# Causal scores of a retention layer on the four quarters of the array, by half chunks

## Chip, cores and metric

One core of a Trainium2 chip runs the whole program. The metric is the device time of one execution in microseconds (us), the median of several executions.

## What is computed

Retention over q, k, v of shape (4, 8, 576, 64), in float32, followed by two dense layers over the 2304 tokens. Only the first part is touched:

```python
scores = scale * np.matmul(q, k.transpose(0, 1, 3, 2))
gamma = 1.0 - 2.0 ** (-5.0 - np.arange(H, dtype=np.float32))
rel = pos[:, None] - pos[None, :]
Dmat = np.where(rel >= 0, gamma[:, None, None] ** rel[None, :, :], 0.0)
ret = scores * Dmat[None, :, :, :]
return np.matmul(ret, v).astype(np.float32)
```

The first layer is h = x @ w_in (512 to 2048), a quadratic gate, g @ w_out (2048 to 512); the second is (x @ w_a) * (x @ w_b) (512 to 1536), then @ w_out.

## The kernel before

**Units.** Retention runs over 16 units (UNITS), each one batch and one pair of heads. A unit's 576 positions are four full chunks of 128 (FULL) and a tail of 64 (TAIL). Inside a chunk the scores are computed and weighted by a mask; what lies before the chunk comes in through a state of 64 x 64 per head, carried from chunk to chunk. The two heads of a pair lie on partitions 0 to 63 and 64 to 127.

**TensorE per unit n, in this order.** `scores(n)` (line 415): group 1 (the tail and chunks 3 and 2, into `score_b`), then group 0 (chunks 1 and 0, into `score_a`). For each chunk and head it is one matmul with 64 rows of contraction, the 128 keys of the chunk stationary and its 128 queries moving; the tail has 64 and 64. Both tensors have one PSUM bank for each head. The output has the keys on its partitions and the queries along the bank. `key_values(n)` (line 428): eight matmuls of 128 rows, 64 stationary and 64 moving columns, into `kv_b`. Then, for the unit before, `inner(n - 1)` (line 445, masked scores times v, 128 rows, 64 stationary columns) and `across(n - 1)` (line 459, state times decayed queries, 64 rows and 64 stationary columns), both into `ret_b`. Behind unit 15's scores and key-values and unit 14's inner and across comes `hidden(0, 0)` (lines 477 to 479), the first matmuls of the dense layer; it waits for unit 15's masked scores, since it writes the banks of `score_a`. Unit 15's inner and across follow it.

**The other engines per unit.** VectorE (DVE): `decay_mask(n)` multiplies the scores by the mask (lines 607, 609) into `probs`, `state_steps(n)` forms the states (621, 624). In units 8 to 11 it then takes a split of x (633), in units 13, 14 and 15 one of `w1` blocks 0, 1 and 2 (638), each behind a rounding by ScalarE (ACT, 830 and 834). ACT copies `ret_b` to `x_all` (818), and the rounding of `w1` block n - 13 stands ahead of the copy for unit n - 1. GpSimd (POOL): line 389 multiplies the keys by their decay, which `key_values(n)` waits for; lines 396 and 400 decay the queries, behind across of unit n - 2.

**Loads.** All on SyncE's queue: for each unit `kq` (keys and queries, features on partitions, 576 KB), `kvt` (keys and values, tokens on partitions, 512 KB), `vtail` (32 KB), into four slots (SLOTS). `kq` of unit n waits for the scores of unit n - 4, `kvt` for its inner. Behind units 0, 1 and 2 stands the table `decays` of the next pair, that of pair 0 is on ACT's queue. The table has for each pair of heads CONST = 2*128 + 128 + 2 + 1 = 387 floats per partition: mask, decay of the queries, decay of the keys, decay of a chunk. The sixteen blocks of `w1` (512 KB each) follow: block 0 behind unit 12, 1 to 9 behind unit 15, 10 to 15 when retention is done.

Of the kernel before, what the change touches and what calls it, by code (L numbers as in the profile page):

```python
# [24 lines left out]
ALU = mybir.AluOpType  # L25
# [4 lines left out]
P = 128  # L30
# [4 lines left out]
PAIRS = HEADS // 2  # L35
UNITS = BATCH * PAIRS
FULL = SEQ // P
TAIL = SEQ - FULL * P
# [22 lines left out]
SLOTS = 4  # L61
EARLY = 3
W1A = 10
MASKS = 2 * P
CONST = MASKS + P + 2 + 1

# [4 lines left out]
def build(nc, k_q, kv_tok, v_tail, w1, w2_ab, w2_out, decays_c, out):  # L73
    ctx = ExitStack()
    with ctx:
        def sem(name):
            return ctx.enter_context(nc.semaphore(name))

        def sb(name, shape, dt=F32, where=ctx):
            return where.enter_context(nc.sbuf_tensor(name, shape, dt))  # L80

        half = sb("half", [P, 2])
# [11 lines left out]
        with ExitStack() as first:  # L94
# [11 lines left out]
            with ExitStack() as s:  # L106
                kq = sb("kq", [P, SLOTS, 2, SEQ], F32, s)
# [3 lines left out]
                probs = sb("probs", [P, 2, 2, SEQ], F32, s)  # L111
                state = sb("state", [P, 2, FULL, HD], F32, s)
                decays = sb("decays", [P, PAIRS, CONST], F32, s)
            with ExitStack() as s:
# [33 lines left out]
        def ps(name, shape):  # L148
            return ctx.enter_context(nc.psum_tensor(name, shape, F32))

        score_a, score_b = ps("score_a", [P, 2, 512]), ps("score_b", [P, 2, 512])
# [20 lines left out]
        wo_loaded = [sem(f"wo_loaded{i}") for i in range(2)]  # L172
        halves_set = sem("halves_set")
        tails_zeroed = sem("tails_zeroed")
        keys_decayed = sem("keys_decayed")
        q_ready = sem("q_ready")
        scores_ready = sem("scores_ready")
        kv_ready = sem("kv_ready")
        probs_ready = sem("probs_ready")
# [53 lines left out]
        def groups(g):  # L233

            if g == 0:
                return [(0, P, 0), (1, P, P)]
            return [(2, P, 0), (3, P, P), (4, TAIL, 2 * P)]

        def width(g):
            return 2 * P if g == 0 else 2 * P + TAIL  # L240
# [14 lines left out]
        def o_rows(n):  # L255

            q, a = n // ROWS, n % ROWS
            at = (q // (NF2 // GROUP)) * SUPER + a * P
            return x_all[:, :, at:at + P]
# [26 lines left out]
        def scores_of(g):  # L286
            return score_a if g == 0 else score_b
# [90 lines left out]
        @block.gpsimd  # L378
        def _(pool):
            nc.gpsimd.memset(half[:, 0:1], 0.5).then_inc(halves_set, 1)  # L380
            nc.gpsimd.memset(half[:, 1:2], -0.5).then_inc(halves_set, 1)
            for n in range(UNITS):
                s, p, r = n % SLOTS, n % PAIRS, n // SLOTS + 1
                if n < PAIRS:
                    pool.wait_ge(decays_loaded[p], 16)
                pool.wait_ge(kvt_loaded[s], 16 * r)
                keys = kvt[:, s, 0, :, :].rearrange("p c (h d) -> p c h d", h=2)
                kdec = decays[:, p:p + 1, MASKS + P:MASKS + P + 2]
                nc.gpsimd.tensor_tensor(keys, keys, kdec.unsqueeze(3).to_broadcast([P, FULL, 2, HD]),
                                        ALU.mult).then_inc(keys_decayed, 1)  # L390
                pool.wait_ge(kq_loaded[s], 16 * r)
                if n >= 2:
                    pool.wait_ge(ret_ready, 2 * (n - 1))

                qdec = decays[:, p, MASKS:MASKS + P]
                nc.gpsimd.tensor_tensor(
                    qd[:, n % 2, P:FULL * P].rearrange("p (c i) -> p c i", c=FULL - 1),
                    kq[:, s, 1, P:FULL * P].rearrange("p (c i) -> p c i", c=FULL - 1),
                    qdec.unsqueeze(1).to_broadcast([P, FULL - 1, P]), ALU.mult)
                nc.gpsimd.tensor_tensor(qd[:, n % 2, FULL * P:], kq[:, s, 1, FULL * P:],  # L400
                                        qdec[:, 0:TAIL], ALU.mult).then_inc(q_ready, 1)

        @block.tensor
        def _(pe):
            def scores(n):
                s = n % SLOTS
                pe.wait_ge(kq_loaded[s], 16 * (n // SLOTS + 1))
                for g in (1, 0):
                    if n:
                        pe.wait_ge(probs_ready, 3 * (n - 1) + (3 if g == 0 else 2))  # L410

                    for c, ln, at in reversed(groups(g)):
                        for head in range(2):
                            dims = slice(head * HD, (head + 1) * HD)
                            mm = pe.matmul(scores_of(g)[0:ln, head, at:at + ln],
                                           kq[dims, s, 0, c * P:c * P + ln],
                                           kq[dims, s, 1, c * P:c * P + ln], start=True, stop=True)
                    mm.then_inc(scores_ready, 1)

            def key_values(n):  # L420
# [11 lines left out]
            def inner(n):  # L432
                s = n % SLOTS
                pe.wait_ge(vtail_loaded[s], 16 * (n // SLOTS + 1))
                if n == 0:
                    pe.wait_ge(tails_zeroed, 2)
                pe.wait_ge(probs_ready, 3 * n + 3)
                for g in range(2):
                    if n:
                        pe.wait_ge(ret_copied, 2 * (n - 1) + g + 1)  # L440
                    for c, ln, at in groups(g):
                        for head in range(2):
                            dims = slice(head * HD, (head + 1) * HD)
                            v = kvt[:, s, 1, c, dims] if c < FULL else vtail[:, s, dims]
                            mm = pe.matmul(ret_b[g][dims, at:at + ln], v,
                                           probs[:, n % 2, head, c * P:c * P + ln],
                                           start=(at == 0), stop=(c == 0), skip_group_check=True)
                mm.then_inc(inner_done, 1)
# [51 lines left out]
            for n in range(UNITS):  # L500
                scores(n)
                key_values(n)
                if n:
                    inner(n - 1)
                    across(n - 1)
# [88 lines left out]
        def _(dve):  # L594
            def decay_mask(n):
                p = n % PAIRS
                if n < PAIRS:
                    dve.wait_ge(decays_loaded[p], 16)
                mask = decays[:, p, 0:MASKS].rearrange("p (h i) -> p h i", h=2)
                for g in (1, 0):  # L600
                    dve.wait_ge(scores_ready, 2 * n + 2 - g)
                    if n >= 2:
                        dve.wait_ge(inner_done, n - 1)
                    o = probs[:, n % 2, :, 2 * g * P:2 * (g + 1) * P].rearrange("p h (c i) -> p h c i", c=2)
                    i = scores_of(g)[:, :, 0:2 * P].rearrange("p h (c i) -> p h c i", c=2)
                    m = mask.unsqueeze(2).to_broadcast([P, 2, 2, P])
                    nc.vector.tensor_tensor(o, i, m, ALU.mult).then_inc(probs_ready, 1)
                    if g:
                        nc.vector.tensor_tensor(probs[0:TAIL, n % 2, :, FULL * P:],
                                                score_b[0:TAIL, :, 2 * P:2 * P + TAIL],  # L610
                                                mask[0:TAIL, :, 0:TAIL], ALU.mult).then_inc(probs_ready, 1)

            def state_steps(n):
# [4 lines left out]
                for c in range(FULL):  # L618
# [3 lines left out]
                    else:  # L622
                        dve.wait_ge(state_ready, FULL * n + c)
                        nc.vector.scalar_tensor_tensor(
                            out=state[:, n % 2, c, :], in0=state[:, n % 2, c - 1, :],
                            scalar=decays[:, p, CONST - 1:CONST], in1=kv, op0=ALU.mult,
                            op1=ALU.add).then_inc(state_ready, 1)
# [61 lines left out]
            def add_rows(step, place):  # L689
                for n in shares_ended(step, place):  # L690
                    if not first_share(n):
                        dve.wait_ge(rows_done, n + 1)
                        nc.vector.tensor_tensor(o_rows(n), y_b[n % 4].rearrange("p (k i) -> p k i", k=KT),
                                                o_rows(n), ALU.add).then_inc(rows_out[n % 4], 1)


            nc.vector.memset(vtail[TAIL:, :, :], 0.0).then_inc(tails_zeroed, 1)
            nc.vector.memset(probs[TAIL:, :, :, FULL * P:], 0.0).then_inc(tails_zeroed, 1)
# [277 lines left out]
def constants():  # L976
    heads = np.arange(HEADS, dtype=np.float32)
    gamma = (1.0 - 2.0 ** (-5.0 - heads)).astype(np.float64)
    pos = np.arange(P, dtype=np.float64)

    rel = pos.reshape(1, 1, 1, P) - pos.reshape(P, 1, 1, 1)
    mask = np.where(rel >= 0, gamma.reshape(1, PAIRS, 2, 1) ** np.maximum(rel, 0), 0.0) / np.sqrt(HD)
    rows = np.repeat(gamma.reshape(PAIRS, 2), HD, axis=1).T
    qdec = rows[:, :, None] ** pos[None, None, :] / np.sqrt(HD)
    kdec = gamma.reshape(1, PAIRS, 2) ** (P - pos)[:, None, None]
    gchunk = rows[:, :, None] ** P
    return np.concatenate([mask.reshape(P, PAIRS, MASKS), qdec, kdec, gchunk], axis=2).astype(np.float32)


# [42 lines left out]
```

## Time and profile before

| | us |
|---|---|
| median of 3 executions | 881.88 (881.67 to 882.44) |
| the profiled execution | 882.61 |
| its span, first to last instruction | 880.1 |
| PE busy | 870.2 (99%) |
| DVE busy | 479.8 (55%) |
| ACT busy | 334.6 (38%) |
| POOL busy | 37.0 (4%) |

PE stands for TensorE's matmuls, PEld for its weight loads, which run beside them. A profile page begins with the busy time of each engine and then cuts the span into 40 slices of 22 us, one digit each, the busy share in tenths. In a timeline, a row is a run of like instructions: start, time from the first one's start to the last one's end, engine, line, operation, output and input, rows*columns of the stationary operand for PE, shapes, count, and in brackets how long the engine had been idle and what ended that. A matmul's own duration contains its way through the array; several lie over each other, so their pace is read from the spacing of the starts: (length of the row - duration of one) / steps. Retention lies in the first 70 us or so.

### The profile page before, as it was taken

How to read it: one execution, taken by the hardware profiler on the slowest of the kernel's cores; microseconds unless marked ns; L12 is line 12 of the kernel's file. 1: busy time of each engine (PE TensorE's matmuls, PEld its weight loads, DVE VectorE, ACT ScalarE, POOL GpSimd, SP SyncE). 2: the span in 40 equal slices, each digit the busy share in tenths (PEclk: the TensorE clock that was granted, in tenths of full speed). 3: DMA queues.
4: the chain of work that ended last, by engine and by line, in shares of the span. 5: the costliest groups of instructions: out<-in, count | busy, mean ns of one | idle time of the engine just before them, and what ended most of it. 6: DMA issues, size and time to landing. Idle time of an engine off the chain costs nothing.

```text
span 880.1 us, 13001 instructions
## 1 busy us (share of the span) xinstructions
PE 870.2 (99%) x5232; PEld 777.0 (88%) x5232; DVE 479.8 (55%) x829; ACT 334.6 (38%) x598; POOL 37.0 (4%) x54
## 2 busy tenths in 40 slices
PE   7999999999999999999999999999999999999998
PEld 6998888888899888888889999999999999999996
DVE  4686665555656755665653533574433574534443
ACT  1235554444445544444443333342233242223220
POOL 4660000000000000000000000000000000000000
PEclk9999999999999999999999999999999999999999
DMA  9996000223232123222335644545454845454622
GB/s 344 329 348 264 1 0 1 79 111 116 111 123 108 54 107 119 111 112 105 118 149 189 243 168 184 198 157 200 150 198 157 284 159 215 168 216 168 227 60 72
DMA packets 33451, 136.89 MB, mean 156 GB/s; under 512 B 2672, under 2 KB 13424, under 8 KB 28784
## 3 DMA queue, kind: packets, MB, share of 16 engines
q1 hardware_dynamic: 33248, 135.87, 42.0%
q8 instruction: 41, 0.67, 0.3%
q10 hardware_dynamic: 144, 0.20, 0.1%
q14 instruction: 18, 0.15, 0.0%
HBM read 109.32 MB, written 26.74 MB: 155 GB/s over the span
## 4 chain that ended last, share of the span: by engine, by line
PE 97%; DMA 1%; SPq 1%; DVE 0%; ACT 0%; issue 0%; POOL 0%; POOLq 0%; DVEq 0%; ACTq 0%
PE score_b L523 6%; PE score_b L527 6%; PE score_b L525 6%; PE score_a L527 4%; PE score_a L523 4%; PE score_a L525 4%; PE score_a L477 4%; PE kv_b L494 4%; PE kv_b L496 4%; PE score_a L479 4%; PE ret_b L496 4%; PE score_b L479 4%; PE score_a L478 4%; PE kv_b L495 4%; PE score_b L477 4%; PE ret_b L495 4%
## 5 line engine op out<-in xcount | busy, mean ns | idle before, releaser
L717 DVE TENSOR_TENSOR gate_w<-relu_s,relu_r 128x512 f32<-128x512 f32 (+1 forms) x80 | 51.0, 638 | 97.2 <-ACT relu_r L895 97.1
L523 PE MATMUL score_b<-xop_hi,wop 128*128 128x384 f32 x288 | 96.8, 336 | 0.1
L527 PE MATMUL score_b<-xop_hi,wop 128*128 128x384 f32 x288 | 96.7, 336 | 0.0
L525 PE MATMUL score_b<-xop_lo,wop 128*128 128x384 f32 x288 | 96.5, 335 | 0.0
L904 ACT ACTIVATE gh<-gated 128x512 fp32r<-128x512 f32 (+1 forms) x80 | 47.2, 590 | 105.9 <-DVE gated L720 105.9
L726 DVE TENSOR_TENSOR gl<-gated,gh 128x512 fp32r<-128x512 f32 (+1 forms) x80 | 51.1, 639 | 50.8 <-ACT gh L904 50.6
L523 PE MATMUL score_a<-xop_hi,wop 128*128 128x384 f32 x216 | 72.2, 334 | 0.0
L527 PE MATMUL score_a<-xop_hi,wop 128*128 128x384 f32 x216 | 72.2, 334 | 0.0
L525 PE MATMUL score_a<-xop_lo,wop 128*128 128x384 f32 x216 | 72.2, 334 | 0.0
L954 ACT ACTIVATE p<-score_b 128x384 f32<-128x384 f32 x36 | 17.7, 490 | 105.3 <-PE score_b L527 105.3
L523 PEld LDWEIGHTS score_b<-xop_hi,wop 128*128 128x128 f32 x288 | 54.1, 188 | 2.0 <-ACT p L954 0.4
L946 ACT ACTIVATE ph<-prod 128x384 fp32r<-128x384 f32 x36 | 18.9, 526 | 96.4 <-DVE prod L763 96.4
L525 PEld LDWEIGHTS score_b<-xop_lo,wop 128*128 128x128 f32 x288 | 54.1, 188 | 1.3
L527 PEld LDWEIGHTS score_b<-xop_hi,wop 128*128 128x128 f32 x288 | 54.0, 188 | 0.0
L720 DVE SCALAR_TENSOR_TENSOR gated<-relu_s,gate_w 128x512 f32<-128x512 f32 (+1 forms) x80 | 51.1, 638 | 2.7
L781 DVE TENSOR_TENSOR prod<-score_a,a 128x384 f32<-128x384 f32 x18 | 10.0, 557 | 72.6 <-PE score_a L527 72.6
L893 ACT ACTIVATE relu_s<-score_a,half 128x512 f32<-128x512 f32 (+1 forms) x40 | 25.8, 646 | 55.4 <-PE score_a L479 55.4
L781 DVE TENSOR_TENSOR prod<-score_b,a 128x384 f32<-128x384 f32 x18 | 10.0, 557 | 64.5 <-PE score_b L527 64.5
L477 PE MATMUL score_a<-xh,w1a 128*128 128x512 f32 (+1 forms) x120 | 44.4, 370 | 0.0
L478 PE MATMUL score_a<-xl,w1a 128*128 128x512 f32 (+1 forms) x120 | 44.2, 368 | 0.0
L479 PE MATMUL score_a<-xh,w1a 128*128 128x512 f32 (+1 forms) x120 | 44.1, 368 | 0.0
L548 PE MATMUL kv_b<-wo_hi,pl 128*128 128x512 f32 x112 | 43.9, 392 | 0.0
(129 smaller groups left out, 2144.1 us busy)
## 6 DMA issues: line engine op xcount, KB each, us to landing
wop<-w_ops SPq DMA_DIRECT2D x36, 1792.0 KB, 7.2
w_ops<-op_hi SPq DMA_DIRECT2D x12, 896.0 KB, 4.7
w_ops<-op_lo SPq DMA_DIRECT2D x12, 896.0 KB, 6.5
kq<-k_q SPq DMA_DIRECT2D x16, 576.0 KB, 6.2
wo_raw<-w_out SPq DMA_DIRECT2D x9, 1024.0 KB, 9.6
kvt<-kv_tok SPq DMA_DIRECT2D x16, 512.0 KB, 5.7
ab_raw<-w_ab SPq DMA_DIRECT2D x12, 512.0 KB, 3.7
w1a_raw<-w SPq DMA_DIRECT2D x10, 512.0 KB, 10.1
```

The costliest lines, as they stand in the source:

```text
L477: pe.matmul(o, w1_slab(f, 0)[:, at], xh[:, k, 0:WIDTHS[t]], start=(k == 0), stop=False)
L478: pe.matmul(o, w1_slab(f, 0)[:, at], xl[:, k, 0:WIDTHS[t]], start=False, stop=False)
L479: mm = pe.matmul(o, w1_slab(f, 1)[:, at], xh[:, k, 0:WIDTHS[t]], start=False, stop=(k == KT - 1))
L495: pe.matmul(o, w1_slab(f, 0)[:, at], gl[:, f % RING, 0:WIDTHS[t]], start=False, stop=False)
L496: mm = pe.matmul(o, w1_slab(f, 1)[:, at], gh[:, f % RING, 0:WIDTHS[t]], start=False, stop=(f == NF1 - 1))
L523: pe.matmul(o, w[:, 0, at], xop_hi[b][:, k, :], start=(start and k == 0), stop=False, skip_group_check=True)
L525: pe.matmul(o, w[:, 0, at], xop_lo[b][:, k, :], start=False, stop=False, skip_group_check=True)
L527: mm = pe.matmul(o, w[:, 1, at], xop_hi[b][:, k, :], start=False, stop=(k == 1), skip_group_check=True)
L717: nc.vector.tensor_tensor(gate_w[:, 0:WIDTHS[t]], relu_s[:, 0:WIDTHS[t]], relu_r[:, 0:WIDTHS[t]], ALU.add).then_inc(gatew_ready, 1)
L720: nc.vector.scalar_tensor_tensor(out=gated[:, 0:WIDTHS[t]], in0=relu_s[:, 0:WIDTHS[t]], scalar=1.0, in1=gate_w[:, 0:WIDTHS[t]], op0=ALU.mi ...
L726: nc.vector.tensor_tensor(gl[:, f % RING, 0:WIDTHS[t]], gated[:, 0:WIDTHS[t]], raw(gh[:, f % RING, 0:WIDTHS[t]]), ALU.subtract).then_inc(g ...
L904: nc.scalar.activation(gh[:, f % RING, 0:WIDTHS[t]], gated[:, 0:WIDTHS[t]], ACT.Copy).then_inc(gh_ready, 1)
```

## The change

The scores of a chunk are computed by halves of 64 keys. The first half meets all 128 queries of the chunk, the second half only the last 64, for the quarter of the square that is left has all its keys behind its queries and is masked out. So each chunk and head has a matmul of 64 stationary and 128 moving columns and one of 64 and 64. A half goes to output partitions 0 to 63 or 64 to 127; in odd chunks the two halves change places (`half_at`), so that the four matmuls of two neighbouring chunks and two heads lie on four different quarters of the array: row half by head, column half by chunk. The order in a group is: the tail (group 1), then the first halves of both chunks, then the second halves of both.

Since the keys of odd chunks now lie swapped on the partitions of the scores, the host swaps the halves of odd chunks in `kvt` (keys and values), and the table holds the mask a second time with its halves swapped and a key decay for each chunk: 4*128 + 128 + 8 + 1 = 649 floats per partition and pair. VectorE's mask product takes the doubled mask as it lies, without a broadcast over chunks. The part of `score_a` and `score_b` that no matmul writes any more is zeroed once at the start by two memsets on VectorE, for which the first scores and the first mask product wait.

```diff
-MASKS = 2 * P
-CONST = MASKS + P + 2 + 1
+HP = P // 2
+MASKS = 4 * P
+KDEC = MASKS + P
+CONST = KDEC + 2 * FULL + 1
@@
+        def half_at(c, half):
+            return HP * (half ^ (c % 2))
@@ (GpSimd)
-                kdec = decays[:, p:p + 1, MASKS + P:MASKS + P + 2]
+                kdec = decays[:, p, KDEC:KDEC + 2 * FULL].rearrange("p (c h) -> p c h", c=FULL)
@@ (TensorE)
+                if n == 0:
+                    pe.wait_ge(scores_zeroed, 2)
                 for g in (1, 0):
                     if n:
                         pe.wait_ge(probs_ready, 3 * (n - 1) + (3 if g == 0 else 2))
-                    for c, ln, at in reversed(groups(g)):
+                    def part(c, half, at, ln):
+                        rows, first = slice(half_at(c, half), half_at(c, half) + HP), c * P + half * HP
                         for head in range(2):
                             dims = slice(head * HD, (head + 1) * HD)
-                            mm = pe.matmul(scores_of(g)[0:ln, head, at:at + ln],
-                                           kq[dims, s, 0, c * P:c * P + ln],
-                                           kq[dims, s, 1, c * P:c * P + ln], start=True, stop=True)
+                            mm = pe.matmul(scores_of(g)[rows, head, at + half * HP:at + half * HP + ln],
+                                           kq[dims, s, 0, first:first + HP], kq[dims, s, 1, first:first + ln],
+                                           start=True, stop=True)
+                        return mm
+                    if g:
+                        part(FULL, 0, 2 * P, TAIL)
+                    for half in range(2):
+                        for c, ln, at in groups(g)[:2]:
+                            mm = part(c, half, at, P - half * HP)
                     mm.then_inc(scores_ready, 1)
@@ (VectorE)
+                if n == 0:
+                    dve.wait_ge(scores_zeroed, 2)
-                    o = probs[:, n % 2, :, 2 * g * P:2 * (g + 1) * P].rearrange("p h (c i) -> p h c i", c=2)
-                    i = scores_of(g)[:, :, 0:2 * P].rearrange("p h (c i) -> p h c i", c=2)
-                    m = mask.unsqueeze(2).to_broadcast([P, 2, 2, P])
-                    nc.vector.tensor_tensor(o, i, m, ALU.mult).then_inc(probs_ready, 1)
+                    nc.vector.tensor_tensor(probs[:, n % 2, :, 2 * g * P:2 * (g + 1) * P],
+                                            scores_of(g)[:, :, 0:2 * P], mask,
+                                            ALU.mult).then_inc(probs_ready, 1)
@@
+            nc.vector.memset(score_b[:, :, 0:2 * P], 0.0).then_inc(scores_zeroed, 1)
+            nc.vector.memset(score_a[:, :, 0:2 * P], 0.0).then_inc(scores_zeroed, 1)
@@ (host)
+    mask = np.stack([mask, halves_swapped(mask, 0)], axis=3)
+    kdec = np.stack([halves_swapped(kdec, 0) if c % 2 else kdec for c in range(FULL)], axis=2)
@@
-        return token_major(a)[:, :FULL * P].reshape(UNITS, FULL, P, P).transpose(0, 2, 1, 3)
+        chunks = token_major(a)[:, :FULL * P].reshape(UNITS, FULL, P, P)
+        chunks = [halves_swapped(chunks[:, c], 1) if c % 2 else chunks[:, c] for c in range(FULL)]
+        return np.stack(chunks, axis=2)
```

## Rows read from the trace of the kernel before

**Rows 1.** The page: busy time of the engines, and the chain's shares.

```profile
PE 870.2 (99%) x5232; PEld 777.0 (88%) x5232; DVE 479.8 (55%) x829; ACT 334.6 (38%) x598; POOL 37.0 (4%) x54
...
PE 97%; DMA 1%; SPq 1%; DVE 0%; ACT 0%; issue 0%; POOL 0%; POOLq 0%; DVEq 0%; ACTq 0%
```

**Rows 2.** Waits, 0 to 92 us: us in total, times, longest us.

```profile
PE score_b L415 <- DMA kq<-k_q: 5.6, 1, 5.6
...
POOL kvt L389 <- DMA kvt<-kv_tok: 13.2, 7, 6.3
...
PEld kv_b L428 <- POOL kvt L389: 1.2, 3, 0.5
```

**Rows 3.** DMA, 0 to 80 us in 40 slices of 2 us; the table's queue.

```profile
DMA  1899999999999997899899899999998999953999
GB/s 25 261 409 400 381 399 364 405 362 378 398 374 362 387 308 249 293 364 312 312 336 320 294 340 333 380 385 363 312 282 310 420 404 420 416 207 55 367 416 416
...
q10 hardware_dynamic: 144, 0.20, 0.8%
```

**Rows 4.** Timeline, 30 to 42 us: one steady unit, PE and PEld.

```profile
33.40 0.92 PE L415 MATMUL score_b<-kq 64*64 64x64 f32 x11
...
34.16 0.61 PE L415 MATMUL score_a<-kq 64*128 64x128 f32 x8
...
34.70 0.55 PEld L428 LDWEIGHTS kv_b<-kvt 128*64 128x64 f32 x16
...
35.21 1.05 PE L445 MATMUL ret_b<-probs,kvt 128*64 128x128 f32 x16
...
37.02 0.27 PE L415 MATMUL score_b<-kq 64*64 64x64 f32 x1
37.02 0.27 PE L459 MATMUL ret_b<-qd,state 64*64 64x64 f32 x3
...
37.12 0.92 PE L415 MATMUL score_b<-kq 64*64 64x64 f32 x11
```

**Rows 5.** Timelines from 0 and (Pool's) from 18 us: key products, one key-value run.

```profile
7.12 1.04 POOL L389 TENSOR_TENSOR kvt<-kvt,decays 128x512 f32<-128x512 f32 x1 [6.26 <-DMA kvt<-kv_tok]
...
14.22 1.04 POOL L389 TENSOR_TENSOR kvt<-kvt,decays 128x512 f32<-128x512 f32 x1 [1.22 <-DMA kvt<-kv_tok]
...
18.71 1.04 POOL L389 TENSOR_TENSOR kvt<-kvt,decays 128x512 f32<-128x512 f32 x1 [2.38 <-DMA kvt<-kv_tok]
...
19.81 0.69 PE L428 MATMUL kv_b<-kvt 128*64 128x64 f32 x16 [0.27 <-POOL kvt L389]
...
21.67 1.04 POOL L389 TENSOR_TENSOR kvt<-kvt,decays 128x512 f32<-128x512 f32 x1 [0.84 <-DMA kvt<-kv_tok]
...
24.68 1.06 POOL L389 TENSOR_TENSOR kvt<-kvt,decays 128x512 f32<-128x512 f32 x1 [0.73 <-DMA kvt<-kv_tok]
...
28.03 1.04 POOL L389 TENSOR_TENSOR kvt<-kvt,decays 128x512 f32<-128x512 f32 x1 [0.47 <-DMA kvt<-kv_tok]
```

**Rows 6.** Single lines' instructions, 33 to 37 us: duration ns min/median/max.

```profile
L415 PE MATMUL score_a<-kq x8: 272/272/272, 34.2 to 34.5; 64*128 64x128 f32 x8
...
L428 PEld LDWEIGHTS kv_b<-kvt x16: 132/138/138, 34.7 to 35.1; 128*64 128x64 f32 x16
```

**Rows 7.** Timeline, 44 to 82 us: where retention ends.

```profile
45.54 0.69 DVE L607 TENSOR_TENSOR probs<-score_b,decays 128x512 f32<-128x512 f32 x1 [0.57 <-PE score_b L415]
...
62.17 1.06 ACT L834 ACTIVATE w1a<-w1a_raw 128x1024 fp32r<-128x1024 f32 x1 [2.06 <-DMA w1a_raw<-w]
...
63.13 0.70 ACT L818 ACTIVATE x_all<-ret_b 128x256 f32<-128x256 f32 x2
...
65.00 1.22 PE L445 MATMUL ret_b<-probs,kvt 128*64 128x128 f32 x15
...
65.20 0.67 DVE L607 TENSOR_TENSOR probs<-score_a,decays 128x512 f32<-128x512 f32 x1
...
67.30 0.50 PE L477 MATMUL score_a<-xh,w1a 128*128 128x512 f32 x1
```

More of the change, by code:

```diff
@@ L174, in build @@
         tails_zeroed = sem("tails_zeroed")
+        scores_zeroed = sem("scores_zeroed")
         keys_decayed = sem("keys_decayed")
@@ L985, in constants, with halves_swapped @@
     kdec = gamma.reshape(1, PAIRS, 2) ** (P - pos)[:, None, None]
+    kdec = np.stack([halves_swapped(kdec, 0) if c % 2 else kdec for c in range(FULL)], axis=2)
     gchunk = rows[:, :, None] ** P
-    return np.concatenate([mask.reshape(P, PAIRS, MASKS), qdec, kdec, gchunk], axis=2).astype(np.float32)
+    parts = [mask.reshape(P, PAIRS, MASKS), qdec, kdec.reshape(P, PAIRS, 2 * FULL), gchunk]
+    return np.concatenate(parts, axis=2).astype(np.float32)
+def halves_swapped(a, axis):
+    return np.roll(a, HP, axis=axis)
 def kernel(q, k, v, moe_w_in, moe_w_out, moe2_w_a, moe2_w_b, moe2_w_out):
```

## The prediction

> **What bounds the kernel now.** I read the page first: TensorE (PE) is busy 870.2 of 880.1 us and carries 97% of the chain [rows 1]. So time is won only where PE's own work shrinks, and only if nothing else then holds PE. The list of waits of the first 92 us, in which all of retention lies, says how far away the others are: PE waits 5.6 us for the first `kq`, and PE's weight loads wait only 1.2 us for Pool's decayed keys. Pool itself waits 13.2 us for `kvt` transfers [rows 2]. The two-microsecond slices show why: the DMA moves 360 to 400 GB/s from the fourth microsecond on and its share stands at nine tenths nearly throughout retention [rows 3]. So two resources lie close together: PE needs 3.72 us per unit (the tail's scores start at 33.40 and at 37.12) [rows 4], and the DMA brought the `kvt` of units 4 and 5 3.01 us apart [rows 5].
>
> **Part 1, scores on four quarters.** A float32 matmul leaves two records (`score_a` in one unit: 4 matmuls, x8) [rows 6]. The eight `score_a` records, 0.27 each, start over 0.61 - 0.27 = 0.34 us, three steps of 0.113: two records (two heads) per step, for 128 moving columns. The key-value records, 64 moving columns, take (0.55 - 0.14) / 7 = 0.059 per pair of weight loads; 128 columns behind 64 stationary ones (inner) take (1.05 - 0.27) / 7 = 0.111 per pair [rows 4, 6].
> Before, from the tail's start at 33.40 to `score_a` at 34.16 is 0.76: tail 2 x 0.059 = 0.12, chunks 4 x 0.113 = 0.45, and 0.19 left over. From 34.16 to the inner matmuls at 35.21 is 1.05: 4 x 0.113 + 8 x 0.059 = 0.92, leaving 0.13. From 35.21 to 37.12 is 1.91: inner 8 x 0.111 + 2 x 0.059, across 6 x 0.111 + 2 x 0.059 = 1.79, leaving 0.12. These three remainders stand exactly where the shape on the array changes (64x64 to 64x128, 64x128 to 128x64, 128x64 to 64x64); between across and the tail's scores, both 64x64, there is none, and one tail record even starts together with the last across records, at 37.02 [rows 4]. I price a change of shape at 0.19 for the one that goes.
> The Trainium skill (TensorEngine Tiling (Array Packing), Key Properties) says that changing the tiling mode, unlike changing the tile, drains the engine. The remainders agree.
> After, all scores are 64x64, so the change between the tail and the chunks goes: -0.19. Per group a chunk is one half of 128 columns and one of 64, and two chunks x two heads fill four quarters. If four records go side by side at the pace at which two do, a group takes 2 x 0.111 + 2 x 0.059 = 0.34 instead of 0.45: -0.11, twice per unit. Sum 0.19 + 0.22 = 0.41 per unit; I take 0.40.
> What speaks for four at once: at 37.02 a record of `score_b` (row half 64, column half 0) starts beside across records on the two diagonal quarters, so three quarters run together (the quarters of the across heads are taken, the record can only be the tail's other head), and a later instruction overtakes earlier ones of an occupied quarter [rows 4]. Each head writes its own bank, as before.
> From the other side: instructions. The scores go from 10 matmuls (20 records) to 18 (36). The closest spacing held over a stretch is the key-value one, 0.029 per record; at that pace 36 records take 1.06 against 0.79 by columns, and the saving shrinks to 0.12 + 0.90 + 0.19 - 1.06 = 0.15 per unit. The bounds of part 1 by these rows are 0.15 and 0.42, and a loss only by the mechanism under rivals.
>
> **Part 2, the table of decays grows** from 387 to 649 floats per partition: a head pair's transfer from 198 to 332 KB. Pair 0's goes on ACT's queue, 1 to 3 stand on SP's queue, each ahead of its unit's `kq` and `kvt`. All four lie before unit 3's keys. The landings show the price: Pool starts on units 0 and 2 at 7.12 and 14.22, 3.55 per unit (with a table of 198 KB), on 4 and 5 at 21.67 and 24.68, 3.01 apart (without) [rows 5]. So 198 KB cost 0.54, and 134 KB more 0.36; by the bytes of table queue 10 (0.20 MB in 0.8% of 80 us) [rows 3] it is 0.43, at the 380 GB/s of the slices 0.35. Four times: +1.4 us (1.2 to 1.7) on the landing of unit 3's keys, 18.71 -> 20.1; Pool's product takes 1.04, so its key-value matmuls start at 21.2 instead of 19.81 [rows 5]. PE comes earlier than that (unit 2's keys land at about 15.2, kv at 16.3, plus 3.3), so the saving of the first units is lost in this wait and +1.4 stands. Bounds: 1.0 (if the table rows move better in longer pieces) and 1.8.
> Does it go on? Unit 4's keys land at 21.67 + 1.4 = 23.1, ready at 24.2, while PE wants them at 21.2 + 3.32 = 24.5; unit 5's ready at 27.2, wanted at 27.8. From there PE leads again, each key transfer is sent when the unit four before it is through (SP), and at 3.32 us per unit the DMA must move 576 + 512 + 32 KB (1.147 MB), 345 GB/s, below the 380 of the slices. Cover is thin, not gone.
>
> **Part 3, small things.** Two memsets of PSUM on DVE ahead of the others stand where nothing else is queued but the two memsets of before; even at 1 us each (a 128x512 product with a PSUM operand takes 0.69 [rows 7]) they end before the first `kq` lands at 5.6 [rows 2], for which PE and, behind it, DVE wait anyway: 0. DVE's mask product loses its broadcast, same 512 elements per partition, 0.69: 0 +- 0.05, and even in a unit with a split DVE sits idle 0.57 us ahead of it [rows 7]. Pool's key product reads its factor from other addresses: 0. The swapped halves are made on the host: 0.
>
> **Part 4, what meets the earlier PE at the end.** Nothing ahead of unit 15 waits on `w1`, but on ACT the rounding of `w1` block 1 stands before the copy that frees `ret_b` for inner of unit 14, and on DVE its split stands before unit 15's mask, on which the first hidden matmul waits. The transfer landed at 62.17; ACT's copy began at 63.13, was through at about 63.5 (half of the row's 0.70) for inner at 65.00, the mask ended at 65.20 + 0.67 = 65.87 for hidden at 67.30: 1.4 us of slack [rows 7]. PE will be there 12 x 0.40 - 1.4 = 3.4 us earlier; the transfer is sent behind unit 15's keys, which wait for inner of unit 11, some 9 x 0.40 - 1.4 = 2.2 earlier. Slack left 0.2, and the DMA is asked for more per us in units 12 to 15 (one `w1` block beside them). I take +0.4 (0 to 1.5). Later nothing: hidden needs a new block only every 24 matmuls, and they arrive in a row.
>
> **Sum.** 12 steps from unit 3 to unit 15 x -0.40 = -4.8; +1.4; +0.4: **-3.0 us**. The profiled run was 882.61 (span 880.1), it would become 879.6; the median of the runs 881.88 becomes **878.9**.
>
> **Rivals.**
> B, instruction pace. Quarters overlap, but records come no faster than 0.029 each: 0.15 per unit, 12 x 0.15 = 1.8, less 1.4, and no squeeze at the end: 881.5. For it: nothing in retention is issued faster over a stretch. Against: PE's queue has slow stretches (across, inner) in which to get ahead, and starts a few ns apart occur.
> The Trainium skill (TensorE: Matmul & The Clock Gate, "Wait - 56ns, not 53.3ns?") gives some 62 ns of sequencer work per matmul where it is not decoded in hardware. Eighteen matmuls would be 1.12 us, a saving of 0.09 per unit and no gain in total; the rows' eight key-value matmuls in 0.47 us, 59 ns each, don't exclude it.
> C, the DMA becomes the bound: the keys land every 3.5 us instead of 3.3, as between units 2 and 6 (14.22 to 28.03, 3.45 each) [rows 5]. Then 12 x 0.22 - 1.4 = 1.2: 880.7.
> D, slower: not more than two score records run at a time (two streams for the same rows, or weight loads of the second column half waiting). A group is then 4 x 0.111 + 4 x 0.059 = 0.68 instead of 0.45, 0.46 more per unit, less 0.19: 12 x 0.27 + 1.4 = +4.6: 886.5. With -0.19 for the change of shape, the kernel gets slower once a group takes over 0.49 us, by 0.2% at 0.56. Against it: the three at 37.02.
> E, the table costs more than its bytes (a 2.5 us hole before unit 3) with part 1 as forecast: 4.8 - 2.5 - 0.4 = 1.9: 880.0.
>
> **Chances.** Forecast (878 to 880) 0.5, B 0.17, C 0.13, E 0.08, D 0.12. A change under 0.2% (1.8 us) can't be told from none: faster (below 880.1) is the forecast and most of E, some of C: 0.6; same 0.28 (B, most of C); slower 0.12 (D). Range 877.3 (part 1 at its full 0.42 and the lower bounds of the delays: -5.0 + 1.0 = -4.0, and a little) to 882.3 (B with the upper bound of the table); D is left out.
>
> **What would show it.** `score_a` and `score_b` as 64x64 records, four within about 0.03 us, `score_b` to `score_a` near 0.46 and a unit at 3.32 us in the thirties; Pool's product of unit 3 starting near 20.1; PE waiting for it about 1.5 us; the first hidden matmul near 64.3. Wrong if units stay above 3.5 us with PE busy (B, D), if Pool waits for `kvt` beyond unit 6 with PE behind it (C), or if unit 3's keys land as early as before.

## The result and the profile after

| | before | after |
|---|---|---|
| median, us | 881.88 | 886.08 |
| range of the runs (5 each) | 881.52 to 882.73 | 885.97 to 887.3 |
| ratio, 95% interval | | 1.0048 (1.0036 to 1.0059) |
| span of the profiled execution | 880.1 | 884.1 |
| PE busy | 870.2 | 866.7 |

The change makes the kernel 4.2 us slower, while PE is busy 3.5 us less. The page's line of the instruction queue has two fetches more than before (41 there):

```profile
PE 866.7 (98%) x5488; PEld 774.3 (88%) x5488; DVE 481.0 (54%) x831; ACT 334.8 (38%) x598; POOL 36.7 (4%) x54
...
q8 instruction: 43, 0.70, 0.3%
```

The timeline from 30 to 42 us, the stretch of [rows 4], PE alone. Columns as there: start, length, engine, line, operation; in brackets the idle time and what ended it.

```profile
34.47 0.27 PE L426 MATMUL score_b<-kq 64*64 64x64 f32 x1
34.47 0.27 PE L477 MATMUL ret_b<-qd,state 64*64 64x64 f32 x3
...
34.58 0.56 PE L426 MATMUL score_b<-kq 64*64 64x64 f32 x18
...
34.98 0.55 PE L426 MATMUL score_a<-kq 64*64 64x128 f32 x15
...
35.46 0.69 PE L446 MATMUL kv_b<-kvt 128*64 128x64 f32 x16
...
35.97 1.05 PE L463 MATMUL ret_b<-probs,kvt 128*64 128x128 f32 x16
...
37.88 0.56 PE L426 MATMUL score_b<-kq 64*64 64x64 f32 x18
...
38.76 0.69 PE L446 MATMUL kv_b<-kvt 128*64 128x64 f32 x16
...
40.97 1.09 PE L463 MATMUL ret_b<-probs,kvt 128*64 128x128 f32 x16 [1.52 <-issue]
```

The first unit is what part 1 forecast: 34.58 to 37.88 is 3.30 us instead of 3.72. The scores take 0.40 from `score_b` to `score_a` and 0.48 from there to the key-value matmuls, which with 0.13 for the change of shape in it is 0.35 for a group. Fifteen `score_a` records start within 0.55 - 0.22 = 0.33 us, 0.024 apart. So four quarters do work at once. The next unit has a hole: the key-value matmuls start at 38.76, the inner ones not 0.51 later but at 40.97, and what ended the wait is "issue", no engine and no data.

The list of waits, 0 to 92 us, has these lines (before, PE's only wait for issue was 0.5 us on weight loads):

```profile
POOL kvt L396 <- DMA kvt<-kv_tok: 12.5, 7, 6.3
...
PE ret_b L463 <- issue: 3.6, 3, 1.6
...
PE kv_b L446 <- POOL kvt L396: 1.5, 2, 0.8
PE kv_b L446 <- issue: 1.5, 1, 1.5
...
PE score_a L426 <- issue: 1.0, 2, 0.7
```

The start and the end of retention, to be read beside [rows 5] and [rows 7], from the timelines from 0, from 48 and from 60 us:

```profile
11.99 1.12 PE L446 MATMUL kv_b<-kvt 128*64 128x64 f32 x16 [0.79 <-POOL kvt L396]
...
12.90 1.92 PE L463 MATMUL ret_b<-probs,kvt 128*64 128x128 f32 x16
...
14.61 1.04 POOL L396 TENSOR_TENSOR kvt<-kvt,decays 128x512 f32<-128x512 f32 x1 [1.59 <-DMA kvt<-kv_tok]
...
17.43 0.69 PE L446 MATMUL kv_b<-kvt 128*64 128x64 f32 x16
...
19.37 1.05 POOL L396 TENSOR_TENSOR kvt<-kvt,decays 128x512 f32<-128x512 f32 x1 [1.38 <-DMA kvt<-kv_tok]
...
20.73 0.69 PE L446 MATMUL kv_b<-kvt 128*64 128x64 f32 x16
...
24.32 0.34 PE L426 MATMUL score_a<-kq 64*64 64x64 f32 x7 [0.32 <-issue]
...
52.23 0.62 PE L446 MATMUL kv_b<-kvt 128*64 128x64 f32 x14 [1.49 <-issue]
...
62.98 0.55 PE L426 MATMUL score_a<-kq 64*64 64x128 f32 x11 [0.71 <-issue]
...
66.76 0.69 PE L446 MATMUL kv_b<-kvt 128*64 128x64 f32 x16
...
69.67 0.54 PE L463 MATMUL ret_b<-probs,kvt 128*64 128x128 f32 x5 [1.58 <-issue]
...
71.28 0.50 PE L495 MATMUL score_a<-xh,w1a 128*128 128x512 f32 x1
```

**Where the 4.0 us of the span come from.** Unit 3's key-value matmuls start at 20.73 instead of 19.81: +0.9. Twelve units of 3.30 instead of 3.72: -5.0. But from 20.73 to unit 15's at 66.76 it is 46.0 and not 39.6: +6.4. From there to the first hidden matmul it is 4.52 instead of 2.81: +1.7. Sum +4.0, and hidden starts at 71.28 instead of 67.30. After that the two kernels run alike.

**What the +0.9 consists of.** Unit 3's keys land 0.66 us later and are ready at 19.37 + 1.05 = 20.42. Its key-value matmuls start at 20.73 without a wait: 3.30 us behind unit 2's at 17.43. So here PE came last, by 0.3 us, and not the keys. PE was late because it ran slowly until 16.6 us: unit 0's inner matmuls (12.90) take 1.92 us, in the kernel before 1.04 (at 12.54). The trace's first record of a full granted clock stands at 16.60, before at 12.31. The same rows with the same lengths (1.12 and 1.92) come back once in the run phase below, from 70.55 on, where the profile gives a granted clock of 0.50. Ahead of 16.60 PE had waited 0.75 and 0.79 us for keys. Other runs have this first record between 9.17 and 15.57, and why it comes late in one and early in another is open.

**What the holes have in common.** I counted PE's records (weight loads, matmuls, waits) in the order of their starts, and took the packets of queue 8 from the trace, each 16,384 bytes, 256 instructions of 64 bytes. Every hole of the changed kernel from unit 4 on lies right behind record 705, 961, 1473, 1985, 2497 or 2753, all 193 plus a multiple of 256:

```
records   start of   packet that brings   from the start of
before    the next   the next block       the record before
          one, us    (start to end)       to this start, us
 705      24.32      21.78 to 22.81       0.54
 961      29.98      27.39 to 28.46       0.81
1217      34.86      31.57 to 33.15       0.00
1473      40.97      38.68 to 39.65       1.74
1729      46.17      43.06 to 44.07       0.00
1985      52.23      49.97 to 50.93       1.72
2241      57.53      55.19 to 56.30       0.29
2497      62.98      60.40 to 61.42       0.98
2753      69.67      67.16 to 68.10       1.85
```

Where there is a hole, PE goes on 1.2 to 1.6 us after the packet's end. This holds for all eleven traces of this case, the runs below included: between 12 and 75 us no block starts sooner than 1.23 us after the end of its packet, and the 25 gaps of over 0.2 us at block starts all end 1.23 to 1.58 us after it.

Two things differ from the kernel before. Its blocks last 6.5 us (33.30 to 39.71 to 46.22) and none runs dry; a unit has 36 matmuls of four records and some waits before, 44 after, in less time, so a block lasts some 4.7 us. And the packets wait longer now. From the moment a block is entered to the start of the packet for the next one it was 2.6, 1.9, 1.6, 0.8, 0.5 and 4.3 us before (blocks entered from 27.04 to 59.13), and 3.1, 1.6, 3.8, 2.1, 3.8, 3.0 and 2.9 after (24.32 to 57.53). The 4.3 shows how near the kernel before already was to a hole: the packet for the block that starts at 65.74 ran from 63.41 to 64.40, 1.34 before it.

### The profile page after: what moved, and what is told of

It is laid out like the page before. It is cut to its first block, busy times and chain, and to the rows that moved or that the text cites. A ratio compares the mean times of both kernels' runs of the same rounds, so it can differ in the third digit from the quotient of the medians.

```text
span 884.1 us, 13516 instructions
## 1 busy us (share of the span) xinstructions
PE 866.7 (98%) x5488; PEld 774.3 (88%) x5488; DVE 481.0 (54%) x831; ACT 334.8 (38%) x598; POOL 36.7 (4%) x54
## 4 chain that ended last, share of the span: by engine, by line
PE 97%; DMA 1%; issue 1%; SPq 0%; DVE 0%; ACT 0%; POOL 0%; DVEq 0%; ACTq 0%; POOLq 0%
PE score_b L541 6%; PE score_b L545 6%; PE score_b L543 6%; PE score_a L545 4%; PE score_a L543 4%; PE score_a L541 4%; PE score_a L495 4%; PE kv_b L512 4%; PE score_b L495 4%; PE ret_b L512 4%; PE score_a L497 4%; PE score_a L496 4%; PE kv_b L513 4%; PE kv_b L514 4%; PE score_b L496 4%; PE ret_b L513 4%
```

## The experiments

**Theory F**: PE runs out of instructions. A block of 256 is asked for when the one before it is entered; the packet waits beside the transfers of `kq` and `kvt`, which keep the DMA nine tenths busy, and a block now lasts less long than that takes. **Rival G**: instructions come at a pace of their own, whatever the data do. **Rival H**: it has nothing to do with counts; the quarters or a semaphore hold PE.

### Less data, the same instructions: light_loads

```diff
+                w = SEQ if n < SLOTS else P
-                sp.dma_start(kq[:, s, :, :], k_q[n]).then_inc(kq_loaded[s], 16)
+                sp.dma_start(kq[:, s, :, 0:w], k_q[n][:, :, 0:w]).then_inc(kq_loaded[s], 16)
+                c = FULL if n < SLOTS else 1
-                sp.dma_start(kvt[:, s, :, :, :], kv_tok[n]).then_inc(kvt_loaded[s], 16)
+                sp.dma_start(kvt[:, s, :, 0:c, :], kv_tok[n][:, :, 0:c, :]).then_inc(kvt_loaded[s], 16)
```

> The changed kernel, with the transfers of kq and kvt for units 4 to 15 cut to 128 of 576 positions and to one chunk of four (the rest of a slot keeps an older unit's numbers, so those units are not computed rightly); all instructions of all engines stay. Theory F (PE runs out of instructions: their fetches, 256 instructions each, queue behind the data transfers of retention): the holes of 0.4 to 1.7 us in PE at every 256th instruction go between units 4 and 12, units take 3.30 us there, and only the two holes beside the w1 blocks (62.98 and 69.67) may stay; 8.1 us of holes become 0 to 2.6, so 886.1 becomes 878 to 881. Theory G (instructions come at a fixed pace, whatever the data traffic; 45 more of them per us is too many): the holes stay, 886. Theory H (the quarters themselves or a semaphore hold PE): the holes stay, 886.

Measured: 879.23, ratio to before 0.997 (0.9959 to 0.9981), 6.9 us below the changed kernel. Its DMA line from 24 to 56 us, and PE's key-value matmuls from its timeline of PE:

```profile
DMA  5420643051515224535042503406998416410575
...
24.02 0.69 PE L448 MATMUL kv_b<-kvt 128*64 128x64 f32 x16
27.32 0.69 PE L448 MATMUL kv_b<-kvt 128*64 128x64 f32 x16
30.62 0.69 PE L448 MATMUL kv_b<-kvt 128*64 128x64 f32 x16
33.92 0.69 PE L448 MATMUL kv_b<-kvt 128*64 128x64 f32 x16
...
57.04 0.69 PE L448 MATMUL kv_b<-kvt 128*64 128x64 f32 x16
60.34 0.69 PE L448 MATMUL kv_b<-kvt 128*64 128x64 f32 x16
62.55 0.54 PE L465 MATMUL ret_b<-probs,kvt 128*64 128x128 f32 x5 [0.88 <-issue]
```

Twelve units of 3.30 us in a row, with all instructions. The packets of the blocks entered at 28.49, 33.33, 37.69, 42.90 and 47.19 start 0.9, 0.1, 0.6, 0.4 and 1.5 us later; in the changed kernel, between 29.98 and 57.53, it was 1.6, 3.8, 2.1, 3.8, 3.0 and 2.9. The one hole left is at record 2753, beside the `w1` blocks (its packet started 3.7 us after the block was entered). G and H fall: the instructions, the quarters and the semaphores are the same here, and 3.30 us per unit is kept up. What it doesn't show alone is that the boundaries of blocks are the places; the next run does.

### The blocks shifted: phase

```diff
+            for i in range(128):
+                pe.wait_ge(scores_zeroed if i % 2 else halves_set, 1)
             for n in range(UNITS):
                 scores(n)
```

> The changed kernel with 128 waits that are long met ahead of PE's first scores, while PE waits for the first kq anyway. They become some 64 to 127 more instructions. Theory F and G: holes stand at every 256th instruction of PE, so in the program they come 64 to 127 instructions earlier, at other matmuls than before (so far unit 4's score_a, units 6, 9, 12 and 14, behind the 705th, 961st, 1473rd, 1985th, 2497th and 2753rd instruction); counted with the added ones they stand at the same numbers. The sum of the holes may change by some us either way. Theory H: the holes stay at the same matmuls. Time within 883 to 889 by all.

The 128 waits became 64 instructions (two conditions in each). Holes over 0.2 us stood behind records 449 (0.80), 705 (0.40), 961 (2.35), 1473 (0.27), 1729 (2.07), 2241 (1.74) and 2753 (2.93): at the same numbers, 64 instructions earlier in the program. The one at 961 was in inner of unit 4 in the changed kernel, and is now in the last records of the scores of a unit (timeline of PE, 26 to 31 us):

```profile
27.21 0.55 PE L426 MATMUL score_a<-kq 64*64 64x128 f32 x14
29.89 0.27 PE L426 MATMUL score_a<-kq 64*64 64x64 f32 x1 [2.13 <-issue]
30.09 0.69 PE L446 MATMUL kv_b<-kvt 128*64 128x64 f32 x16
```

The one run took 888.97, within the expectation of 883 to 889: another phase, other holes, in sum more. About 1 us of it is not the holes themselves: PE stood from 67.4 to 70.13, the granted clock fell from 1.0 to 0.5 (to 1.2 GHz) at 69.88 and rose again at 73.29, and from unit 15's key-value matmuls to hidden it took 3.80 us instead of 2.81. The waits also held PE's first scores until 8.47 instead of 5.78, and unit 3's key-value matmuls still started at 20.62. Here the clock was full from 11.85, PE came early and waited 0.71 us for unit 3's keys, so in this run their landing decided.

### The w1 blocks later: w1_late

```diff
-            for f in range(1, W1A):
-                load_w1(f)
+            load_w1(1)
+            load_w1(2)
+            sp.wait_ge(ret_ready, 2 * UNITS - 2)
+            for f in range(3, W1A):
+                load_w1(f)
```

> The changed kernel with w1 blocks 3 to 9 sent when unit 14 is through, instead of behind unit 15's keys; nothing computed changes. Theory F: the hole of 1.85 us at 69.67, whose fetch ran from 67.16 beside these transfers, shrinks to under 0.5; the one at 62.98 (0.98) may shrink. 886.1 becomes 883.5 to 884.7. Theories G and H: no change, 886.

Measured: 885.2 (882.45 to 887.34, 6 runs), 1.0031 (1.0015 to 1.0048). The hole at record 2753 is gone (its packet ran from 63.85 to 64.82, PE got there at 66.14) and with it most of the 1.7 us; the only wait for issue after unit 12 is this one, from its timeline of PE, 64 to 70 us:

```profile
65.66 1.13 PE L466 MATMUL ret_b<-probs,kvt 128*64 128x128 f32 x16
...
66.84 0.99 PE L480 MATMUL ret_b<-qd,state 64*64 64x128 f32 x16
68.18 0.47 PE L498 MATMUL score_a<-xh,w1a 128*128 128x512 f32 x1 [0.35 <-issue]
```

The holes at 961, 1473 and 1985 stayed, 1.63, 0.65 and 1.60 in the profiled run. The median lies a little above what was expected and the runs spread by 5 us; that the packets' waits differ from one execution to the next would explain it, but one execution alone was profiled. The medians (885.2 against 886.08) would not carry F.

The 0.35 us at 68.18 does not stand at a block's start. VectorE's mask product for unit 15 (`probs<-score_a`, 67.40, 0.67 us long) ends at 68.07 there, since the 2.05 us split of a `w1` block (64.63) stood ahead of it on VectorE. Hidden waits for this mask: it is the wait that part 4 of the prediction named, and it cost about 0.2 us (3.03 from unit 15's key-value matmuls instead of 2.81).

### The table alone: big_table

```diff
-CONST = MASKS + P + 2 + 1
+CONST = MASKS + P + 2 + 1 + 262
```

> The kernel before, with 262 unused floats added to each partition's table of a head pair, so that it is as long as in the changed kernel. The prediction's part 2 said +1.4 us (bounds 1.0 and 1.8): 883.3. The trace of the changed kernel shows its unit 3 keys landing 0.66 us later (19.37 instead of 18.71), which would make +0.6 to +0.7: 882.5. If the fetches of instructions are slowed by it too, holes appear in PE as well, and it is more.

Measured: 882.87, 1.0012 (1.0003 to 1.0022): +1.0 us. In its timeline unit 3's keys come at 19.61 and its key-value matmuls at 20.89, in the kernel before 18.71 and 19.81:

```profile
19.61 1.06 POOL L389 TENSOR_TENSOR kvt<-kvt,decays 128x512 f32<-128x512 f32 x1 [2.29 <-DMA kvt<-kv_tok]
20.89 0.69 PE L428 MATMUL kv_b<-kvt 128*64 128x64 f32 x16
```

So the landing moves 0.9, PE 1.1, and hidden 0.8 (68.09). PE was 0.2 us behind the keys here too (ready at 20.67; unit 2's key-value matmuls at 17.17 plus 3.72 is 20.89; full clock from 15.37). 134 KB more per unit cost 0.9 / 4 = 0.23 us of landing, less than in proportion to the 0.54 that the first 198 KB seemed to cost. No holes appeared; 3.72 us per unit throughout.

### More instructions in the old scores: more_instructions

```diff
+            def met_waits():
+                pe.wait_ge(tails_zeroed, 1)
+                pe.wait_ge(halves_set, 1)
@@ ahead of each matmul of retention
+                            met_waits()
```

> The kernel before, with its old scores, and ahead of each of a unit's 36 matmuls two waits that are long met: about 36 more instructions of PE per unit, 183 in place of 147, and the same work for the array. Theory F: 256 instructions now last 5.2 us instead of 6.5, less than the 6 to 7 us that a fetch takes from the moment its predecessor is entered; holes of 1 to 2 us appear at every 256th instruction, 4 to 9 us in sum, 886 to 891. Theory H (the holes belong to the quarters): no holes; the units stay at 3.72 us, or all get longer by the same amount if PE's sequencer can't keep up with the waits, at most 1.8 us each.

Inconclusive. The time was 902.62 (one run), a unit took 5.2 us, evenly: 576 met waits (36 in a unit) cost 1.5 us per unit, 0.04 each. So 256 instructions lasted 7 us and there was nothing to see at their boundaries; the largest gap there was 0.13 us. F's figure of 886 to 891 was wrong because I had taken the added instructions as free, and the result is what H allowed in its second branch. A kernel with the old scores and blocks of under 5 us was not measured.

### Fewer transfers under way: capped

As w1_late, and:

```diff
                 if n >= SLOTS:
+                    sp.wait_ge(kvt_loaded[(n - 1) % SLOTS], 16 * ((n - 1) // SLOTS + 1))
                     sp.wait_ge(scores_ready, 2 * (n - SLOTS) + 2)
```

> As w1_late, and kq of a unit from the fourth on is only sent when kvt of the unit before has landed, so that at most one unit's transfers stand ahead of a fetch of instructions. Theory F: fetches start within 2 us instead of 3 to 4 after they are due, the holes at 30, 40 and 52 us shrink below 0.5 each; if the DMA then has pauses, Pool waits for keys instead. 881 to 883, against 885 of w1_late. Theory G: the holes stay, 885.

Measured: 906.82, 1.0285 (1.027 to 1.0301), 25 us slower than before. No wait for issue stood in retention up to 80 us, but PE waited for keys:

```profile
DMA  0469775008999207899508499800999950539992
...
POOL kvt L400 <- DMA kvt<-kv_tok: 47.6, 15, 6.2
...
PE kv_b L450 <- POOL kvt L400: 16.3, 11, 2.6
```

The DMA (24 to 56 us) now has pauses, a unit takes 5 to 6 us. The expectation was off by twenty-odd us: with transfers that take 3.7 (`kq`) and 4.8 us (`kvt`) from issue to landing there, a stream of 3.3 us per unit needs more than one unit under way. The granted clock fell to 0.5 three times as well, for 3.4 us each (from 32.63, 63.35 and 80.42). About F this run says nothing: its blocks lasted 6.5 to 9.1 us between 23.66 and 78.01, as long as in the kernel before or longer.

### The quarters in every other unit, in the last eight, in the last four

every_other is w1_late with the following; even units have the matmuls of the kernel before, and its order of halves on the host:

```diff
                         for c, ln, at in groups(g)[:2]:
+                            if n % 2:
                                 mm = part(c, half, at, P - half * HP)
...
```

> As w1_late, with the quarters in odd units alone; even units have the old scores of 128 keys, and the old order of halves in kvt, mask and key decay. Theory F: a pair of units takes 3.30 + 3.72, and 256 instructions last 5.5 us, nearer to what a fetch takes: holes 0 to 3 us in sum instead of 5, the saving 6 x 0.42 = 2.5 instead of 5.0; 881 to 883. Theory H (the quarters as such): holes only in odd units, 883 to 885.

last_four and last_eight have `n >= Q0` in that place, with Q0 = 12 and 8, and load the table's added part later (at n == 3 in last_eight):

```diff
+                if n == 7:
+                    sp.dma_start(decays[:, :, LATE:], decays_c[:, :, LATE:]).then_inc(late_loaded, 16)
```

> The quarters in units 12 to 15 alone, with the order of halves in kvt, mask and key decay switched there too; the second half of the table (1056 bytes per partition and pair) is sent in one transfer behind unit 7, so the start has the old table of 198 KB; w1 blocks 3 to 9 wait until unit 14 is through, as in w1_late. Theory F: units 12 to 15 meet a DMA that is running empty, so 256 instructions may last less than 5 us there without a hole; 4 x 0.42 = 1.7 us saved, the start as in the kernel before: 880.2 (879.8 to 881). Theory G (a fixed pace of instructions): a hole of 1 to 2 us in units 12 to 15, 881.5 to 882.

> The same from unit 8 on, the second half of the table behind unit 3. Theory F: units 8 to 11 run beside the full DMA, where a fetch takes 6 to 7 us from the moment it is due; 8 x 0.42 = 3.4 us less, one or two holes of 1 to 1.7 us between 40 and 56 us: 879.5 to 881.5. Theory G: three or four holes, 882 to 884.

| | median, us | ratio to before | units after unit 3, us |
|---|---|---|---|
| every_other | 881.74 | 1.0 (0.9991 to 1.001) | 3.72 / 3.30 in turn, once 3.84, 4.14 and 4.49 |
| last_four | 881.6 | 0.9997 (0.9987 to 1.0006) | 3.72, then 3.30, 3.30, 3.30, 4.76 |
| last_eight | 882.74 | 1.0006 (0.9997 to 1.0015) | 3.72, then 3.30, 3.30, 3.69, 3.30, 4.68, 4.09, 3.62, 3.30; unit 4 4.36 |

(The last column is from the starts of the key-value matmuls.) None beats the kernel before by what can be told. The quarters save their 0.42 in each unit that has them, and block boundaries take it back. every_other came out as F expected. last_four (881.6) and last_eight (882.74) did not: both lie where their expectations put theory G, with the hole or holes that it named. It is light_loads that rules G out, not these two; what they show is that I had set the packets' waits too short.

In last_four, where the start has the old table and unit 3's matmuls start at 19.35, one hole remains (timeline of PE from 59 us):

```profile
60.65 0.98 PE L501 MATMUL ret_b<-qd,state 64*64 64x128 f32 x15
62.74 0.21 PE L501 MATMUL ret_b<-qd,state 64*64 64x64 f32 x1 [1.12 <-issue]
```

Its packet ran from 60.28 to 61.30 though its predecessor was entered at 56.14. The claim in its expectation that units 12 to 15 meet a DMA running empty was wrong: the keys of unit 15 and two `w1` blocks were still on their way. In every_other 256 instructions last some 5.5 us (two units have 328 in 3.72 + 3.30); one hole of 1.24 us was left, at record 1985, and one of 0.38 at 1473. In last_eight they are 0.33, 1.33 and 0.84, at 1473, 1729 and 1985.

## Why the prediction was wrong

Forecast 878.9, range 877.3 to 882.3, "faster" 0.6. Measured 886.08.

- **Part 1 (0.40 per unit)** was right, mechanism and size: 3.30 us where 3.32 was said, a group 0.35 where 0.34, the change of shape gone. Twelve units bring 5.0.
- **Part 2 (+1.4 at unit 3)** was mis-sized: the keys landed 0.66 us later in the changed kernel and 0.9 in big_table. The step "so 198 KB cost 0.54, and 134 KB more 0.36" took the cost as proportional to bytes; it measured 0.17 and 0.23. PE's key-value matmuls moved 0.9 and 1.1, since "PE comes earlier than that" failed in these two profiles: PE, at the lower clock until 16.60 and 15.37, came 0.3 and 0.2 us after the keys. In phase, w1_late and light_loads it came early and waited for them, as said. The clock was in no term.
- **Part 2, "Does it go on?"** asked only whether data come in time. They did (Pool waited as long for `kvt`, 12.5 instead of 13.2). It didn't ask what else uses the same DMA. Its 380 GB/s is the rate of the first 28 us; from 28 to 60 us [rows 3] has 249 to 385.
- **The step that failed** is the one that priced the added instructions, "From the other side: instructions". It asked how fast PE can issue them and bounded that by the key-value spacing. It never asked how they come to PE. 256 more matmul records and as many weight loads are two more packets in retention, and each packet has to arrive in 4.7 instead of 6.5 us, and the packets also started later than before. That is 6.4 + 1.7 = 8.1 us of holes (with small shifts in between; the seven gaps of the list alone are 7.9), which no term and no rival had. Why the packets started later, and why by so unequal times, is open. The page showed the queue (q8, 41 packets), and the number of records per packet could have been had from it, roughly: 10,464 matmuls and weight loads in 41 packets is 255, PE's own waits not counted.
- **Part 4 (+0.4)** was not put to the test in the changed kernel: PE came late, not early, to the end of retention. In w1_late its mechanism shows, with about 0.2 us.
- **Part 3** cost nothing, as said: two memsets of 0.48 us each, done at 1.94; the mask product 0.69 as before.
- **Rivals.** D had nearly the measured time (886.5) and is still wrong: its mechanism, that no more than two records run at a time, is refuted by the 3.30 us. B (pace of issue) stood closest in subject, but light_loads issues the same instructions at 3.30 us per unit, and the eighteen score matmuls take 0.88 us (34.58 to 35.46), under B's 1.06 and under the 1.12 named beside it. C, the DMA as the bound, was right that the full DMA is where the gain goes, and wrong about which transfers suffer.

The Trainium skill (Runtime: NRT & Kernel Launch, Instruction fetch mechanics) says that each engine's instructions are refilled in 16 KiB blocks of 256, the next while the current one runs, and that the cost of crossing a boundary is mostly hidden. The trace agrees on size and place. On the cost it agrees for the kernel before and for light_loads (with the one hole named), not for the changed kernel, where the boundaries cost 8.1 us; here the measurement decides.

## What to carry to other kernels

More and smaller instructions on PE have a price that no busy share shows: each 256 of them are a 16 KB transfer that shares the DMA with the data. Before splitting matmuls in a stretch where the DMA is nine tenths busy, divide 256 by the instructions per us of that stretch and compare with the time from entering a block to the end of the next one's packet, plus the 1.2 to 1.6 us that follow; here 6.5 us was just enough and 4.7 was not. The faster kernel's packets waited longer, so a figure from the kernel before is a lower bound. In a trace, waits for "issue" at distances of 256 or 512 records are this; one that stands elsewhere (w1_late at 68.18) is not.

## What the runs showed of the hardware that I had not expected

- Four 64x64 quarters of the array took float32 matmuls side by side: 16 records of a group's `score_a` in 0.35 us, where eight of the 64x128 shape took 0.45.
- Where PE stood at a block's start, the block's first instruction came 4.9 to 6.7 us after its predecessor was entered in the changed kernel (up to 7.2 in phase), while the DMA carried data at nine tenths. Of this 1.0 was the packet and 1.2 to 1.6 came after it. With the DMA four tenths busy (light_loads, 24 to 56 us) the packet started within 0.1 to 1.5 us.
- A wait of PE that is long met cost 0.04 us (more_instructions).
- The granted clock fell from 1.0 to 0.5 at 69.88 us in phase, where PE had stood since 67.4, and was back at 73.29. It first reached 1.0 between 9.17 and 16.60 us, differently in each profile.
- Executions of one kernel differed by 4.9 us in w1_late and by 3.7 in last_four, against 1.9 among 18 executions of the kernel before. Those of the changed kernel (1.3) and of light_loads (1.6) did not differ more than these.
